# Expert tiles of 256 and 128 rows, with weight sets in halves, in a fused RWKV, mixture-of-experts and MLP kernel

## The reference

```python
# 1. linear attention, 8 heads of 48, state carried over 768 steps
y[t] = r[t] @ (state + u*k[t] v[t]);  state = w[t]*state + k[t] v[t]
# 2. mixture of 8 experts, two of them for each token
noisy = x @ w_gate + log1p(exp(x @ w_noise)) * noise
out[token] += weight * (relu(x @ w1[e]) @ w2[e])      # 384 -> 1024 -> 384
# 3. MLP
h = x @ w_in;  out = (h - tanh(h)) @ w_out            # 384 -> 2048 -> 384
```

## Time and profile before

| | |
|---|---|
| median of 3 runs | 1261.28 us (1258.55 to 1262.38) |
| the profiled execution | 1248.69 us, its span 1247.0 us |
| TensorE matmul busy | 1174.9 us (94%) |
| TensorE weight load busy | 1142.7 us (92%) |
| VectorE busy | 717.1 us (58%) |
| ScalarE busy | 537.4 us (43%) |
| expert stage | from 238 to 808 us of the span |
| MLP | from 825 us to the end |

### The profile page before, as it was taken

How to read it: one execution, slowest core, us unless ns; L and a number is a source line. 1 busy time by engine, 2 the same in 40 slices (tenths; PEclk the granted TensorE clock), 3 DMA queues, 4 the chain that set the end, 5 groups by cost and what they waited for, 6 DMA issues and landing times. The chain is left out here.

```text
span 1247.0 us, 25009 instructions
## 1 busy us (share of the span) xinstructions
PE 1174.9 (94%) x9553; PEld 1142.7 (92%) x9553; DVE 717.1 (58%) x1047; ACT 537.4 (43%) x782; POOL 112.5 (9%) x140
## 2 busy tenths in 40 slices
PE   6898978897999999999999999949999999999998
PEld 5787867797999999999999999949999999999998
DVE  7979888748765756576666655523333333343433
ACT  5444533355355555556555555412322322223322
POOL 1000224213100000000000000030101101101010
PEclk8879778699999999999999999969999999999999
DMA  8445445365867777777676656520101101011010
GB/s 166 98 102 106 108 113 171 132 239 196 312 239 245 235 243 249 256 229 255 233 272 218 226 202 241 180 85 1 57 5 53 57 0 57 16 41 57 0 57 19
DMA packets 176523, 179.87 MB, mean 144 GB/s; under 512 B 96816, under 2 KB 159280, under 8 KB 176464
## 3 DMA queue, kind: packets, MB, share of 16 engines
q1 hardware_dynamic: 159152, 146.25, 37.5%
q0 software_dynamic: 6528, 20.06, 4.7%
q10 hardware_dynamic: 10784, 12.78, 2.8%
HBM read 149.18 MB, written 29.88 MB: 144 GB/s over the span
## 5 line engine op out<-in xcount | busy, mean ns | idle before, releaser
L1390 DVE TENSOR_TENSOR w_lo<-w_raw,w_hi 128x1536 fp32r<-128x1536 f32 x126 | 215.9, 1755 | 174.6 <-ACT w_hi L804 174.5
L686 PE MATMUL ps<-xT_hi,w_hi 128*128 128x256 f32 x744 | 213.6, 287 | 8.6 <-DVE xT_lo L1390 4.5
L687 PE MATMUL ps<-xT_lo,w_hi 128*128 128x256 f32 x744 | 212.6, 286 | 0.0
L688 PE MATMUL ps<-xT_hi,w_lo 128*128 128x256 f32 x744 | 212.5, 286 | 0.0
L1390 DVE TENSOR_TENSOR gg<-ps,th 128x768 f32<-128x768 f32 x64 | 61.3, 957 | 234.1 <-ACT th L1003 234.1
L804 ACT ACTIVATE w_hi<-w_raw 128x1536 fp32r<-128x1536 f32 x126 | 180.1, 1478 | 31.9 <-issue 25.0
L704 PE MATMUL ps<-w_hi,h_hi 128*128 128x384 f32 x496 | 168.9, 341 | 1.4 <-DVE h_lo L1468 1.4
L706 PE MATMUL ps<-w_hi,h_lo 128*128 128x384 f32 x496 | 166.2, 335 | 0.0
L705 PE MATMUL ps<-w_lo,h_hi 128*128 128x384 f32 x496 | 165.9, 334 | 0.0
L1003 ACT ACTIVATE th<-ps 128x768 f32<-128x768 f32 x64 | 52.0, 813 | 240.0 <-PE ps L755 240.0
L686 PEld LDWEIGHTS ps<-xT_hi,w_hi 128*128 128x128 f32 x744 | 144.7, 195 | 10.1 <-issue 7.8
(11 more groups left out here) (213 smaller groups left out, 1907.8 us busy)
## 6 DMA issues: line engine op xcount, KB each, us to landing
w_raw<-in_moe_w SPq DMA_DIRECT2D x64, 1536.0 KB, 6.6
xt_in<-xg SPq DMA_DIRECT2D x32, 384.0 KB, 5.1
yg<-y_out ACTq DMA_DIRECT2D x31, 384.0 KB, 4.8
k_pad<-in_k SPq DMA_DIRECT2D x32, 144.0 KB, 3.3
v_nat<-in_v SPq DMA_DIRECT2D x32, 144.0 KB, 3.3
out<-o_out SPq DMA_DIRECT2D x8, 576.0 KB, 4.0
w_nat<-in_w SPq DMA_DIRECT2D x15, 288.0 KB, 3.0
r_pad<-in_r SPq DMA_DIRECT2D x30, 144.0 KB, 2.8
```

The lines of the kernel that those rows point to most:

```text
L686: pe.matmul(o, w1_hi[:, c, cols], xT_hi[:, c, :], start=first, stop=False, skip_group_check=True)
L687: pe.matmul(o, w1_hi[:, c, cols], xT_lo[:, c, :], start=False, stop=False, skip_group_check=True)
L688: mm = pe.matmul(o, w1_lo[:, c, cols], xT_hi[:, c, :], start=False, stop=(c == KD - 1), skip_group_check=True)
L1390: vec.tensor_tensor(dst, a, b, ALU.subtract).then_inc(s, 1)
```

## The change

- The stage gets 20 tiles of 256 rows (`Tile.one` false) and 15 of 128 rows (`one` true): `NPAIR` = 20, `NSING` = 15. The first five tiles are whole ones as before, then tiles of 256 and of 128 alternate. Rows processed fall from 7936 to 7040.
- w1 and w2 are loaded in halves, with a semaphore for each half; the copies, subtractions and matmuls wait for a half. The first half of w2 of the next tile is split at the end of a tile, the second half in the middle of `up`.
- SP works further ahead for x, w1 and w2; the load of a stage is issued in the step of the tile that uses it, behind the w1 loads of the tile after the next.
- The tables get a third part (`late_3`, `late_4`, `first_c`, `shift_c`, `bound_c`), `shifted` two operations more for each expert. The pads behind each region are 128 rows, not 256.
- The loads, transposes and splits for a tile behind the last are gone, and so are the waits for them.

```diff
+NPAIR = (2 * N // TS - E) // 2
+NSING = (2 * N + E * (TS - 1)) // TS - 2 * NPAIR
+NT = NPAIR + NSING
...
-            def tile_loads(i, st):
...
-                reg_wait(sp, xT_full, i + 1)
-                load_x(i + 1)
-                reg_wait(sp, w1_lo_s, 2 * i + 2)
-                load_w1(i + 1)
...
-                reg_wait(sp, w2_lo_s, 2 * i + 2)
-                load_w2(i + 1)
+            def tile_loads(t, second, third, st):
+
+                if second is not None:
+                    reg_wait(sp, w2_lo_s, 2 * t.n + 2)
+                    load_w2(second, 1)
+                if third is not None:
+                    reg_wait(sp, xT_full, t.n + 2)
+                    load_x(third)
+                    for hf in range(2):
+                        reg_wait(sp, w1_lo_s, 2 * t.n + 3 + hf)
+                        load_w1(third, hf)
                 if st is not None:
+                    stage(st)
+                if third is not None:
+                    reg_wait(sp, w2_lo_s, 2 * t.n + 3)
+                    load_w2(third, 0)
...
+            tile_loads(two_parts(0), one_part(0), two_parts(1), 0)
+            tile_loads(one_part(0), two_parts(1), one_part(1), 1)
+            with sp.Fori(1, NSING - 1) as i:
+                tile_loads(two_parts(i), one_part(i), two_parts(i + 1), i + 1)
+                tile_loads(one_part(i), two_parts(i + 1), one_part(i + 1), None)
...
-            def up(i, step=lambda b: None):
+            def up(t, step=lambda b: None):
+
+                w = TS if t.one else T
...
                 for b in range(FC // 2):
-                    pe.wait_ge(h_lo_s, (FC // 2) * i)
+                    if b % 2 == 0:
+                        pe.wait_ge(w1_hi_s, 2 * t.n + 1 + b // 2)
+                        pe.wait_ge(w1_lo_s, 2 * t.n + 1 + b // 2)
+                    pe.wait_ge(h_lo_s, (FC // 2) * t.n)
...
-                            pe.matmul(o, w1_hi[:, c, cols], xT_hi[:, c, :], start=first, stop=False, skip_group_check=True)
+                            pe.matmul(o, w1_hi[:, c, cols], xT_hi[:, c, 0:w], start=first, stop=False, skip_group_check=True)
...
+            with pe.Fori(0, NSING - 1) as i:
+                up(two_parts(i))
+                turn_tile(one_part(i))
+                down(two_parts(i))
+                up(one_part(i))
+                turn_tile(two_parts(i + 1))
+                down(one_part(i))
...
-            def tile_act(i, st, step=lambda k_: None):
-                reg_wait(act, w2_raw_in, 16 * i + 16)
-                after(act, y_full, i)
+            def tile_act(t, nxt, st, step=lambda k_: None):
+                w = TS if t.one else T
+                after(act, y_full, t.n)
                 step(0)
...
                     step(1 + b)
-                w1_high(i + 1)
-                step(5)
-                xT_high(i + 1)
-                step(6)
+                    if b == 1:
+                        w2_high(t, 1)
+                if nxt is not None:
+                    w1_high(nxt, 0)
+                    step(5)
+                    xT_high(nxt)
+                    w1_high(nxt, 1)
+                    step(6)
+                    w2_high(nxt, 0)
                 if st is not None:
                     reg_wait(act, stage_in_s, 16 * st + 16)
...
+                for bound, step in ((bound_b, step_b), (bound_c, step_c)):
+                    seq(vec.tensor_scalar(slot_t[:], slot_f[:], bound[:, e:e + 1], step[:, e:e + 1], ALU.is_ge, ALU.mult))
+                    seq(vec.tensor_tensor(slot_y[:], slot_y[:], slot_t[:], ALU.add))
...
+                       (2, 6): [late[2]], (3, 1): [late[3]], (3, 3): [shifts], (3, 4): [lambda: shifted(0), lambda: shifted(1)],
+                       (3, 6): [lambda: shifted(2), lambda: shifted(3)],
```

More of the change, by code:

```diff
@@ L1 @@
+from collections import namedtuple
 from contextlib import ExitStack
@@ L62, with whole, two_parts, one_part @@
 NA = -(-(2 * 2 * S - E * (T - 1)) // T)
-S0 = NA + 2
+assert NPAIR - NA == NSING and NT <= 39
+Tile = namedtuple("Tile", "one n at xs")
+def whole(k):
+    return Tile(False, k, k, 2 * k)
+def two_parts(i):
+    return Tile(False, NA + 2 * i, NA + i, 2 * NA + 3 * i)
+def one_part(i):
+    return Tile(True, NA + 2 * i + 1, NPAIR + i, 2 * NA + 3 * i + 2)
 def build(nc, r, k, v, w, u, w_gate, w_noise, noise, w1, w2, w_in, w_out, out):
@@ L153, in build @@
         xTr = two(place, "xTr", [P, KD, JH * C])
-        tt = place("tt", [C, 4, 32 * E])
+        tt = place("tt", [C, 3, 24 * E])
         kf = place("kf", [P, TC, D])
@@ L833, in keep_back, with w1_high, w2_high, xT_high @@
                        ps[0:C, TB[half], 0:n * P].rearrange("p (j h d) -> p j h d", h=2, d=HB)[:, :, :, 0:D], T_copied[half])
[L835 to L844, removed]
+            def w1_high(t, hf):
+                reg_wait(act, w1_raw_in[hf], 16 * t.n + 16)
+                follow(act, h_full, (FC // 2) * t.n - (2 if hf == 0 else 0))
+                cols = slice(hf * F // 2, (hf + 1) * F // 2)
+                cp(w1_hi[:, :, cols], w1_raw[:, :, cols], w1_hi_s)
+            def w2_high(t, hf):
+                reg_wait(act, w2_raw_in[hf], 16 * t.n + 16)
+                after(act, (y_half, y_full)[hf], t.n)
+                rows = slice(hf * FC // 2, (hf + 1) * FC // 2)
+                cp(w2_hi[:, rows, :], w2_raw[:, rows, :], w2_hi_s)
+            def xT_high(t):
+                reg_wait(act, xT_full, t.n + 1)
+                if t.one:
+                    cp(xT_hi[:, :, 0:TS], ps[:, 0, 0:KD * TS].rearrange("p (c t) -> p c t", c=KD), xT_hi_s)
+                else:
+                    cp(xT_hi[:, 0:2, :].rearrange("p c t -> p (c t)"), ps[:, 0, :], xT_hi_s)
+                    cp(xT_hi[:, 2, :], ps[:, XB[2], 0:T], xT_hi_s)
             def spread_in(n):
@@ L1386, in tokens, with w1_low, w2_low @@
                                   bv[:].rearrange("t q h d -> t h q d"), ALU.add).then_inc(x_done, 1)
[L1388 removed]
+            early_1, early_2, counts, late, shifts, shifted, slots_final = tables(v_)
             def sub(dst, a, b, s):
                 vec.tensor_tensor(dst, a, b, ALU.subtract).then_inc(s, 1)
[L1392 to L1396 removed]
+            def w1_low(t, hf):
+                cols = slice(hf * F // 2, (hf + 1) * F // 2)
+                v_.wait_ge(w1_hi_s, 2 * t.n + hf + 1)
+                sub(w1_lo[:, :, cols], w1_raw[:, :, cols], w1_hi[:, :, cols], w1_lo_s)
+            def w2_low(t, hf):
+                rows = slice(hf * FC // 2, (hf + 1) * FC // 2)
+                v_.wait_ge(w2_hi_s, 2 * t.n + hf + 1)
+                sub(w2_lo[:, rows, :], w2_raw[:, rows, :], w2_hi[:, rows, :], w2_lo_s)
             take, softplus_1, softplus_2, softplus_3, choose_1, choose_2, weights, placed = router(v_)
```

363 lines of the change are left out of this document (199 added, 164 removed).

## The result

The kernel after takes 1289.0 us (1286.8 to 1293.6), the kernel before 1261.8 in the same session: a ratio of 1.0225, 95% interval [1.0192, 1.0259]. Measured again later the ratio is 1.0246 [1.0188, 1.0303]. The change costs 27 us. The prediction had 1264 in a range of 1254 to 1290, as a kernel that hardly changes. The time is that of its rival "stage load later" (1280, up to 1293).

The account below looks back on a forecast made before the run. TensorE's own time was taken as the bound of the expert stage. Pairs -6.1, waits +3.7, first pair +3.1, early +2.3, end -0.7 give +2.3: 1248.7 to 1251.0, plus 12.6 to the median, say 1264; range 1254 to 1290.

Parts of the forecast that it names:

- stage load later: Rival, pairs of tiles: stage load lands 1.1 us later than reckoned, 1280, or 1293 with its old 6.0; chance 0.25.
- Pace of `up` of B: `up` matmuls of the 128-row tile: weight load sets 0.112 us each, 72 of them 8.06 us.
- four passes: Rival, `up` of the 128-row tile: 128 columns take four passes, 0.224 us a matmul, 1385 us; chance 0.06.
- TensorE's pair: TensorE's time for one 256-row and one 128-row tile without waits: 17.30 + 12.89 = 30.19 us, 15 pairs 452.3.
- Landing of the stage load: Stage load in the 256-row tile: issued 16.5 us into the pair, 4.0 to land, landed at 20.5.
- The chain behind: ScalarE and VectorE work from the stage load's landing to the next `up`: 9.9 us.
- the threshold: Stage load in a pair: no wait if it lands by 20.3 us, 2.1 a pair if it keeps its 6.0.
- B's own stage: First pair's 128-row tile has a stage step too; its `down` begins about 3.1 us late, once: +3.1.
- Early part: Stretch before tile 5: added VectorE table work against gains from w1 halves, tile 5 at 351.9 for 349.58: +2.3 us.
- Base: Whole kernel before: profiled execution 1248.7 us, with the median of the runs 12.6 us above it.
- the stage in A: Stage wait in the 256-row tile of each pair: 0.25 us a pair together with `xT_lo`, 3.7 in all.

Follow-up runs that it names:

- stage_free: Kernel after with stage copies moved to the 128-row tiles, the first pair included, and the sixteenth stage handled behind the last pair: 1259.2 us, ratio 0.9997 to before.
- stage_earlier: Kernel after with SyncE issuing the stage load ahead of the second half of w1 instead of behind it: 1242.7 us, ratio 0.9994 to before.
- stage_later: Kernel after with stage copies and subtractions moved from the 256-row to the 128-row tile in all pairs but the first: 1263.8 us, ratio 1.0029 to before.
- table_later: stage_free with two `shifted` steps and `slots_final` moved from tiles 3 and 4 into the first pair's 256-row tile: 1239.7 us, ratio 0.9962 to before.
- four_widths: Probe on 128-row tiles: the four banks of `up` multiply 128, 64, 192 and 256 columns instead of 128 each; no kernel time or ratio given.
- four_widths_2: Probe like four_widths, with 192, 160, 256 and 128 columns in the four banks; no kernel time or ratio given.

## Why the prediction was wrong

It had the mechanism and the place, and mis-sized one term: the landing of the stage load.

1. **Pace of `up` of B: right.** 0.112 was taken from matmuls with 48 and 8 columns, and 0.1109 is measured. One reading on the way was wrong: the two records of a `scores` matmul cover 0.112 together, not 2 x 0.112. In the trace of before such pairs start 0.112 us apart at clock 1.00, and 0.213 at 0.50. So the trace had a row with 128 columns at just this pace, and "four passes" had less for it than 0.06 says. The Trainium skill (TensorE: Matmul & The Clock Gate, LDWEIGHTS) has the load take the number of weight columns divided by 1.2 in ns, an estimated 107 ns for 128. The traces here agree within 4 ns at granted clock 1.00, and have 0.213 at 0.50. The 81 ns that the Trainium skill gives for a pair of weight load and matmul (same page, Back-to-back issue gap) is not what these matmuls do.
2. **TensorE's pair: nearly right.** 30.19 was forecast without waits, and 30.58 is measured once the stage is gone. Of the excess, 0.34 stand ahead of `up` of A, which begins 0.47 behind the end of `xT_lo` there, just as in the kernel after, where the view names `xT_lo` as the wait. It is even with TensorE, as was said. But the forecast had put 3.7 us for this and the stage load together, and this alone takes 4.9: 457.2 us for the 15 pairs of stage_free against 452.3.
3. **Landing of the stage load: the step that failed.** The prediction has it issued at 16.5, in the queue "a half is in front, about 2.2 us of data left against 4.5, so 4.0: landed at 20.5". The issue was right (16.4). From there it took 5.0 to 6.4 us, 5.7 at the median of pairs 3 to 14: landed at 22.1. More than one half was in front, since the first was not through when the stage was issued. Even with just one half in front, in stage_earlier, it took 4.6 and not 4.0. The chain behind was nearly right, 9.9 reckoned from the landing and 10.3 measured, and so was the threshold: 20.3 in the forecast, 30.58 - 10.3 = 20.3 in the runs. The landing was 1.8 us over it, and 1.8 a pair was lost. The forecast wrote 0.25 for this and `xT_lo` together.
4. **B's own stage: right in kind.** +3.1 was reckoned once, 4.1 measured, in the second pair of stage_later.
5. **Early part: +2.3 reckoned, +0.1 to 0.8 measured** for tiles 1 to 4 (85.5 against 84.8 to 85.4). The halves give back 5.0 us in tiles 1 and 2, and VectorE's table work takes 5.8 in tiles 3 and 4; table_later shows 2.4 us of the latter.
6. **Base.** The sum was made on one execution and moved up by 12.6 us to the median. That was sound: the median of before beside the kernel after was 1261.8.

The account of the error: the 15 pairs were forecast at 452.3 + 3.7 + 3.1 = 459.1 us and took 485.4, 26 more. Of the 33 us above 452.3, 4.9 are item 2, 24 the stage in A and 4.1 B's own stage. The early part took some 2 us less than forecast, which leaves about the 25 us of the miss.

The chances: "stage load later" had 0.25 and is what happened. The wait was seen to be even with TensorE with a landing time guessed to half a us; with such a threshold the likelier side was a loss, as an early landing gives nothing back.

## What to carry to other kernels

When a step is moved in a DMA queue, count the bytes of every transfer that is in front at that moment, and take the landing time of the nearest row until a run shows a shorter one; a load that is wanted in the tile in which it is issued closes a loop around all engines. A wait with a threshold costs nothing below it, and above it every us past the threshold, so a forecast at the threshold should lean to the loss, and the cure can be one issue moved. In these traces fewer columns for each weight load saved nothing from 192 down to 64; what saved time was fewer weight loads, once the order on the engine that paid for it was right.

## What the runs showed of the hardware

A matmul of this type with its own 128x128 weights takes 0.111 to 0.112 us for 64, 128, 160 and 192 columns at granted clock 1.00, 0.120 for 256 (after, four_widths, four_widths_2); at 0.50 192 and 256 columns both take 0.213. In 7 of 15 tiles B the clock fell to 0.50 at or right behind 18 matmuls of 64 columns though TensorE never idled there, in 8 it did not, and never in `up` with 128 columns in all four banks. Why in some and not in others is open.

The load of `stage_in`, 0.2 MB, landed 4.4 to 5.9 us after its issue with one half of w1 (0.79 MB) just ahead of it, 4.8 to 6.9 with two (after, stage_later), 5.7 to 6.8 with a whole w1 set issued 1.2 us ahead, and 2.8 behind the last tile of stage_free, where no load of weights was in front.

The MLP's 413 or 422 us for the same code, by session, stays unexplained; so does tile 0's 22.4 to 30.0.
